# Linear attention and two feed-forward layers: the down, up and second down products as seven half-size block products each

## What is computed

```python
def _attn_ref(q, k, v):                       # q, k, v: (8, 8, 576, 64)
    q_s = softmax(q, axis=-1)                 # each with + 1e-09 under the sum
    k_s = softmax(k, axis=2)
    kv = np.einsum('bhsd,bhse->bhde', k_s, v)
    return np.einsum('bhsd,bhde->bhse', q_s, kv)

# x: attention's output as 4608 tokens x 512
def _moe_ref(x, w_gate, w_val, w_out):        # d_ff 1536
    g = x @ w_gate
    return (g * (1 / (1 + np.exp(-g))) * (x @ w_val)) @ w_out

def _moe2_ref(x, w_in, w_out):                # d_ff 2048; this w_out is w_out2 in the kernel
    h = x @ w_in
    g = np.where(h > 0.0, h, np.exp(np.minimum(h, 0.0)) - 1.0)
    return g @ w_out
```

## Time and profile before

| what | value |
|---|---|
| median of three runs | 1824.34 us |
| span of the profiled execution | 1820.5 us |
| TensorE busy | 1797.6 us, 99% of the span |
| VectorE busy | 763.9 us, 42% |
| ScalarE busy | 562.7 us, 31% |
| GpSimd busy | 131.6 us, 7% |
| mean granted TensorE clock | 0.998 of full speed |

### The profile page before, as it was taken

One profiled execution on the slowest core, in us unless ns is written; L12 is line 12 of the kernel. 1 busy time (PEld: TensorE's weight loads), 2 busy tenths in 40 slices (PEclk: granted clock), 3 DMA queues, 4 the chain that ended last, 5 costly groups with the idle time before them and its releaser, 6 DMA issues.

```text
span 1820.5 us, 21697 instructions
## 1 busy us (share of the span) xinstructions
PE 1797.6 (99%) x8156; PEld 1480.3 (81%) x8156; DVE 763.9 (42%) x1276; ACT 562.7 (31%) x846; POOL 131.6 (7%) x78
## 2 busy tenths in 40 slices
PE   7899999999999999999999999999999999999999
PEld 5688888888888888888888788888888888888887
DVE  6764544545355453542122434343434343433333
ACT  4333333333333333332121223232323232322222
POOL 6800000000000000000007400000000000000000
PEclk9999999999999999999999999999999999999999
DMA  7613121131311313112022301010101010101000
GB/s 216 171 34 95 55 78 50 34 94 55 95 34 34 94 55 101 27 34 76 1 73 89 115 1 46 0 46 0 46 0 46 0 46 0 46 0 46 0 23 23
DMA packets 122421, 94.67 MB, mean 52 GB/s; under 512 B 59936, under 2 KB 96800, under 8 KB 122400
## 3 DMA queue, kind: packets, MB, share of 16 engines
q1 hardware_dynamic: 113424, 76.57, 14.3%
q10 hardware_dynamic: 8976, 17.83, 2.8%
HBM read 66.06 MB, written 28.31 MB: 52 GB/s over the span
## 4 chain that ended last, share of the span: by engine, by line
PE 96%; DVE 3%; issue 1%; ACT 0%; SPq 0%; DMA 0%; DVEq 0%; ACTq 0%
PE psum L537 31%; PE psum L539 30%; PE psum L538 30%; PE psum L492 2%; PE psum L501 1%; PE psum L483 0%; DVE x_lo L812 0%; PE psum L502 0%; DVE k_rowmax L740 0%; DVE x_lo L829 0%; DVE hid_lo L848 0%; DVE q_negmax L746 0%; DVE hid L845 0%; DVE k L776 0%; ACT hid_hi L686 0%
## 5 line engine op out<-in xcount | busy, mean ns | idle before, releaser
L537 PE MATMUL psum<-x_hi,weights 128*128 128x512 f32 x1440 | 569.8, 396 | 5.6 <-DVE x_lo L812 3.5
L539 PE MATMUL psum<-x_lo,weights 128*128 128x512 f32 x1440 | 562.5, 391 | 0.0
L538 PE MATMUL psum<-x_hi,weights 128*128 128x512 f32 x1440 | 561.9, 390 | 0.0
L537 PEld LDWEIGHTS psum<-x_hi,weights 128*128 128x128 f32 x1440 | 271.1, 188 | 65.3 <-DVE x_lo L812 4.3
L539 PEld LDWEIGHTS psum<-x_lo,weights 128*128 128x128 f32 x1440 | 271.1, 188 | 57.6
L538 PEld LDWEIGHTS psum<-x_hi,weights 128*128 128x128 f32 x1440 | 271.3, 188 | 53.9
L537 PE MATMUL psum<-weights,hid_hi 128*128 128x512 f32 x576 | 224.1, 389 | 0.0
L538 PE MATMUL psum<-weights,hid_lo 128*128 128x512 f32 x576 | 224.1, 389 | 0.0
L539 PE MATMUL psum<-weights,hid_hi 128*128 128x512 f32 x576 | 224.1, 389 | 0.0
L845 DVE TENSOR_TENSOR hid<-psum,act_out 128x512 f32<-128x512 f32 x108 | 74.6, 691 | 351.4 <-PE psum L539 323.7
L862 DVE TENSOR_SCALAR act_out<-act_out 128x512 f32<-128x512 f32 x144 | 61.5, 427 | 362.9 <-ACT act_out L702 362.4
(11 more groups left out here) (75 smaller groups left out, 1467.9 us busy)
## 6 DMA issues: line engine op xcount, KB each, us to landing
attention_out_T<-ek_x SPq DMA_DIRECT2D x32, 288.0 KB, 2.2
layer_out_T<-stage ACTq DMA_DIRECT2D x9, 1024.0 KB, 5.0
stage<-layer_out_T SPq DMA_DIRECT2D x9, 1024.0 KB, 5.1
k<-in_k_dram SPq DMA_DIRECT2D x32, 256.0 KB, 2.7
q<-in_q_dram SPq DMA_DIRECT2D x32, 256.0 KB, 2.8
v<-in_v_dram SPq DMA_DIRECT2D x64, 128.0 KB, 2.8
stage<-attention_out_T SPq DMA_DIRECT2D x8, 1024.0 KB, 5.2
out_dram<-stage ACTq DMA_DIRECT2D x8, 1024.0 KB, 4.4
```

Of the source, the lines that this page charges most:

```text
L537: pe.matmul(acc, w_hi, xh, start=start, stop=False)
L538: pe.matmul(acc, w_lo, xh, start=False, stop=False)
L539: return pe.matmul(acc, w_hi, xl, start=False, stop=stop)
```

## The change

The program becomes four stages with their rows in DRAM between. Stage A is gate and value with attention, stage B is w_out, stage C is w_in, and stage D is w_out2. Stage A still works on nine chunks of 512 tokens, with 24 passes per tile and no down product; it stores the hidden rows. Attention's pairs are 6 slots apart instead of 7, and alternate between two pairs of banks.

Stages B, C and D cut weights and rows into 2x2 blocks and form each block product by seven products instead of eight, with added and subtracted blocks (the Winograd variant of Strassen's form: blocks A11, A12, A22 and sums S1 to S4 of the weights). The tokens go in five pairs of halves, of 480, 480, 448, 448 and 448 columns. Per pair B makes 7 forms x 2 output tiles x 6 contraction tiles x 3 passes = 252 passes, C makes 336 in four groups, and D makes 336. GpSimd makes the weight forms in 22 units during stage A, and stores them to DRAM, from which each stage loads its own. It also makes the sums of the rows in B and D (`sum_blocks`), and in C the sums and all `lo` halves of the rows (`split_y`). VectorE makes the `lo` halves in B and D, adds partial products (`add_parts`, `add_u`), does ELU in C (`elu`) and turns D's output in 32x32 blocks, which is then stored in runs of 128 bytes. A ring of 12 split tiles serves B (two forms of 6) and one of 8 serves D (one form of 8).

```diff
+    NX = 480
+    halves = [480, 480, 448, 448, 448]
+    pairs_of_tokens = []
+    at = 0
+    for n in halves:
+        pairs_of_tokens.append((at, n))
+        at += 2 * n
+    assert at == T and max(halves) == NX
+    NP = len(halves)
+    KT1, KT2, KTD = J1 // 2, J2 // 2, KD // 2
+    MW = DM // 2
...
+            def free_for(self, engine, p, i, kt):
+                t = self.seq(p, i, kt) - self.ring
+                if t >= 0:
+                    engine.wait_ge(self.p_done, t // self.kt * (self.kt + 1) + t % self.kt + 2)
...
+            for u in range(len(units)):
+                pool.wait_ge(fact_landed, (u + 1) * 64)
+                pool.tensor_tensor(form(F_S1), form(7), form(F_A22), ALU.add).then_inc(fact_step, 1)
+                pool.tensor_tensor(form(F_S3), form(F_A11), form(7), ALU.subtract).then_inc(fact_step, 1)
+                pool.wait_ge(fact_step, u * 5 + 1)
+                pool.tensor_tensor(form(F_S2), form(F_S1), form(F_A11), ALU.subtract).then_inc(fact_step, 1)
+                pool.wait_ge(fact_step, u * 5 + 3)
+                pool.tensor_tensor(form(F_S4), form(F_A12), form(F_S2), ALU.subtract).then_inc(fact_step, 1)
+                if u:
+                    pool.wait_ge(fact_stored, stores_of(u) * 16)
+                pool.wait_ge(fact_step, u * 5 + 4)
+                pool.tensor_scalar(fact_forms[:, 0, :, :], fact_raw[:, 0:7, :], 1.0, 1.0, ALU.mult, ALU.mult
+                                   ).then_inc(fact_step, 1)
+                pool.wait_ge(fact_step, u * 5 + 5)
+                pool.tensor_tensor(fact_forms[:, 1, :, :], fact_raw[:, 0:7, :], fact_forms[:, 0, :, :].bitcast(F32),
...
+            def sum_blocks(of, p):
+                _, n = pairs_of_tokens[p]
+                r11, r21, r12, r22 = of.slots(p)
+                def chunk(slot, c):
+                    return of.block(slot, n)[:, c * of.chunk:(c + 1) * of.chunk, :]
+                for c in range(of.chunks):
+                    pool.wait_ge(of.raw_landed[r11], 16 * (p + 1))
+                    pool.wait_ge(of.raw_landed[r12], 16 * (p + 1))
+                    pool.tensor_tensor(chunk(r12, c), chunk(r12, c), chunk(r11, c), ALU.subtract).then_inc(of.t_made, 1)
...
+                    pool.wait_ge(of.raw_landed[r22], 16 * (p + 1))
+                    pool.wait_ge(of.lo_made, of.seq(p, 3, (c + 1) * of.chunk - 1) + 1)
+                    pool.wait_ge(of.t_made, of.sums(p, 0, c))
+                    pool.tensor_tensor(chunk(r22, c), chunk(r22, c), chunk(r12, c), ALU.subtract).then_inc(of.t_made, 1)
...
+            def rest_of_y(p, i):
+                _, n = pairs_of_tokens[p]
+                pool.wait_ge(y_hi_made, 7 * p + i + 1)
+                pool.tensor_tensor(c_block(c_lo[i], n), y_source(p, i, n), c_block(c_hi[i], n).bitcast(F32),
+                                   ALU.subtract).then_inc(y_lo_made, 1)
+            def split_y(p):
+                sum_y(p, 0)
+                sum_y(p, 1)
+                rest_of_y(p, 0)
+                sum_y(p, 2)
+                rest_of_y(p, 1)
+                sum_y(p, 3)
+                for i in range(2, 7):
+                    rest_of_y(p, i)
+            for p in range(NP):
+                sum_blocks(stage_b, p)
+            for p in range(NP):
+                split_y(p)
+            for p in range(NP):
+                sum_blocks(stage_d, p)
...
+            def layer1(n):
...
+                    if n == 0:
+                        pe.wait_ge(w_split if j else w0_split, j if j else 1)
+                    if g >= 2:
+                        pe.wait_ge(silu_done, g - 1)
+                    into_hidden(GATE[g % 2], w_g, n, j == 0).then_inc(gate_done, 1)
+                    if n < BA:
                         attend(n, 3 * j)
-                    if j:
-                        pe.wait_ge(h_made, n * J1 + j)
-                    else:
+                    if g == 0:
                         pe.wait_ge(w0_split, 2)
-                    into_hidden(VAL, w_v, n, False).then_inc(val_done, 1)
-                    if with_attention:
+                    if g >= 2:
+                        pe.wait_ge(h_made, g - 1)
+                    into_hidden(VAL[g % 2], w_v, n, False).then_inc(val_done, 1)
+                    if n < BA:
                         attend(n, 3 * j + 1)
-                    if j:
...
+            def down(of, bank, p, i, dp):
+                _, n = pairs_of_tokens[p]
+                w = of.w[i]
+                for kt in range(of.kt):
+                    t = of.seq(p, i, kt)
+                    if dp == 0:
+                        pe.wait_ge(of.lo_made, t + 1)
+                    r = t % of.ring
+                    mm = product(psum[:, bank, 0:n], [w[:, half, kt, dp * P:(dp + 1) * P] for half in range(2)],
+                                 (of.hi[r][:, 0:n], of.lo[r][:, 0:n]),
+                                 kt == 0 and i in (0, 1, 2), kt == of.kt - 1, i > 2)
+                    if dp == 1 or kt == of.kt - 1:
+                        mm.then_inc(of.p_done, 1)
...
+                                    pe.wait_ge(*before[2][dp])
+                            elif i == 3:
+                                bank = 6 + dp
+                                pe.wait_ge(of.p5_copied, u + 1)
+                            else:
+                                bank = dp
+                                pe.wait_ge((of.p1_copied, of.c12_made, of.c22_made)[i - 4], u + 1)
+                            down(of, bank, p, i, dp)
...
+            def rest_of_tile(of, p, i, kt):
+                _, n = pairs_of_tokens[p]
+                t = of.seq(p, i, kt)
+                dve.wait_ge(of.hi_made, t + 1)
+                dve.tensor_tensor(of.lo[t % of.ring][:, 0:n], of.block(of.slot_of(p, i), n)[:, kt, :],
+                                  of.hi[t % of.ring][:, 0:n].bitcast(F32), ALU.subtract).then_inc(of.lo_made, 1)
+            def rest_of_form(of, f):
+                if f < 7 * NP:
+                    for kt in range(of.kt):
+                        rest_of_tile(of, f // 7, f % 7, kt)
...
+            def down_stage(of, part):
+                for f in range(7 * NP):
+                    p, i = divmod(f, 7)
+                    part(p, i, 0)
+                    rest_of_form(of, f + of.ahead)
+                    part(p, i, 1)
...
+            def elu(u, x, at, k):
...
+                e = c_e[x][f][:, side * n:side * n + n]
+                of = psum[:, c_bank(u, x), 0:n] if at == (1, 0) else c_s[x][{(0, 0): 0, (0, 1): 1, (1, 1): 2}[at]][:, 0:n]
+                dve.wait_ge(exped, 2 * u + x + 1)
+                dve.tensor_scalar(e, e, 1.0, 1.0, ALU.min, ALU.subtract).then_inc(m_made, 1)
+                dve.wait_ge(m_made, u * 8 + k + 1)
+                dve.scalar_tensor_tensor(out=e, in0=of, scalar=0.0, in1=e, op0=ALU.max, op1=ALU.add).then_inc(made, 1)
+            def up_stage():
+                for u in range(NP * NG):
+                    if u:
+                        elu(u - 1, 1, (1, 0), 7)
+                    add_u(u, 0, 1)
+                    add_u(u, 1, 1)
+                    elu(u, 0, (0, 0), 0)
+                    elu(u, 1, (0, 0), 1)
+                    add_u(u, 0, 4)
+                    add_u(u, 1, 4)
+                    elu(u, 0, (1, 1), 2)
```

More of the change, by code:

```diff
@@ L38, in attention_two_ffn_kernel @@
     CH = T // C
-    TB = C // P
     HP = H // 2
@@ new lines, in rest_of_x, with beside @@
+            def rest_of_x(n, kd):
+                dve.wait_ge(x_hi_made, n * KD + (kd + 1))
+                dve.tensor_tensor(x_lo[n % 2][:, kd, :], stage[:, kd, :], x_hi[n % 2][:, kd, :].bitcast(F32),
+                                  ALU.subtract).then_inc(x_lo_made, 1)
+            def beside(n, slot):
+                if n < BA:
+                    for hp, step in steps_at(slot - START, STRIDE, STEPS):
+                        for work in steps.get(step, ()):
+                            work(n + 1, hp, False)
+                if n + 1 < CH and slot in X_SLOTS:
+                    rest_of_x(n + 1, X_SLOTS.index(slot))
```

1081 lines of the change are left out of this document (783 added, 298 removed).

## The result

The changed kernel takes 1958.9 us (median of 4 runs, 1956.4 to 1962.0) against 1823.9 us for the kernel before in the same series (1821.9 to 1824.4): ratio 1.074, 95% interval 1.073 to 1.076. It is slower by 135 us, although 132 passes of TensorE are gone and 4620 others are narrower. The forecast was 1906 us, with a range of 1776 to 1985.

What follows compares the result with a forecast made beforehand. TensorE, busy 1797.6 of 1820.5 us, was taken as the bound; 131.4 us less of passes gave 1689.1, and + 50 + 8 + 35 + 24 + 70 + 9 + 17 = 1902.1 profiled, 1906 as median; range 1776 to 1985.

Steps and rivals of the forecast that it cites:

- Pace of the passes: TensorE: passes of 512, 480 and 448 columns take 0.2262, 0.2125 and 0.1987 us, together 131.4 us fewer.
- Stage A: 50 + 8 expected: Stage A: two TensorE waits for each of 28 pairs of heads, 50 us; GpSimd's weight units delaying VectorE, 8 us.
- The second wait: Stage A: turn_q directly behind sum_kv on TensorE waits for VectorE's k_den to kv, 1.2 us a pair of heads.
- The first: Stage A: spread_max directly behind turn_max on TensorE waits for VectorE's k_max, 0.6 us a pair of heads.
- B: 35 expected: Stage B: GpSimd's sums taking turns with VectorE's lo halves delay additions, 7 us a pair, 35 us (bounds 2 and 12 a pair).
- C: 24 expected: Stage C: GpSimd's nine instructions beside each last group delay VectorE, 6 us at each of four crossings, 24 us.
- D: 70 expected: Stage D: GpSimd's burst of sums slows the lo halves of form 4, 14 us a pair, 70 us (bounds 4 and 24).
- Hand-overs and clock: 9 + 17 expected: Three stage changes at 3 us each, 9 us; ten falls of TensorE's clock to 1.2 GHz at 1.7 us, 17 us.
- The base of 1689.1 us: Whole kernel: profiled time if nothing waited, 1820.5 us before less 131.4 us of passes.
- That the turns fit into gaps: Rival for B, C and D: GpSimd's and VectorE's turns mostly cost nothing, so the kernel is faster, 1784 us; chance 0.27.
- The pace set by something other than columns: Rival for TensorE: narrower passes still take 0.2262 us, only 30 us are saved, 2007 us; chance 0.02.
- the second rival: D, C and B at their upper bounds by late sums, 228 us instead of 129, so 2005 us; chance 0.11.

Runs made afterwards that it cites:

- the kernel with both repairs: Changed kernel with attention's second slot ahead of the value block and the sums of B and D made by VectorE: 1759.6 us, ratio 0.965.
- the fillers: Changed kernel with eight more TensorE passes, into a bank nobody reads, ahead of waits for lo tiles in D: 1945.2 us, ratio 1.067.

## Why the prediction was right in kind, and where its sizes were off

The sign and the mechanisms were right, the sum was 53 us short: 1954.7 us profiled against 1902.1. The measured 1958.9 lies in the forecast's 1835 to 1970, near its upper end, and D missed its own sign: 471.4 us where I had put 420 to 440. Step by step, with the stages' times of the profiled executions:

**Pace of the passes: 27 us too low.** This is the step "480 columns take 0.2125 us and 448 take 0.1987". TensorE's timeline of the kernel with VectorE's sums:

```profile
1699.82 0.36 PE L901 MATMUL psum<-g_hi,g_w 128*128 128x448 f32 x1
...
1701.86 0.36 PE L902 MATMUL psum<-g_lo,g_w 128*128 128x448 f32 x1
```

Ten intervals in 2.04 us: 0.204 each and not near the 0.199 that I had asked for; 60 passes of 480 columns from 1180.06 us on start 0.218 apart. D without waits is 353.9 us for 1680 passes, 0.2107 against my 0.2042: 11 us in D, 6 in B (263.1 for 257.3) and, at the same pace, 11 in C. From 512 down to 480 columns a column is worth 0.25 ns, from 480 to 448 0.44: the straight line through 288 and 512 columns gave too much for the first steps down. The Trainium skill's rule in the prediction ("TensorE: Matmul & The Clock Gate", Back-to-back issue gap) has a flatter one: N/2.4 + 2.5 gives 0.189 and 0.2025 us, both below the measured 0.204 and 0.218, so the trace does not bear out its level; its saving, an estimate of 126.9 us, was nearer to what these rows give (131.4 - 27, so about 104) than mine, though still above it.

**Stage A: 50 + 8 expected, 74 us measured** (770.5 against 696.1 without both causes): 62 us for the order of slots, about 9 for the units. The second wait was right: 32.9 / 28 = 1.2 us each, as worked out. The first was 31.1 / 31 = 1.0 rather than 0.6, and the step that failed is "VectorE multiplies `hid` just before, but does so under make_x or sum_kv". VectorE's timeline:

```profile
229.87 0.69 DVE L1445 TENSOR_TENSOR hid<-psum,act_out 128x512 f32<-128x512 f32 x1 [1.95 <-PE psum L933]
230.48 0.28 DVE L1358 TENSOR_REDUCE k_max<-psum 128x1 f32<-128x128 f32 x1
```

The transposition starts at 229.61 directly behind the value block, and so does `hid`; k_max stands behind it in VectorE's list and begins 0.6 us after the transposition has ended (229.61 + 0.27).

**B: 35 expected, 26.5 measured** (289.6 against 263.1 with VectorE's sums). **C: 24 expected, 32 measured** (386.0 against 354 at D's pace), but 10 of the 32 is the store behind the weight loads, which I had bounded as "at most 15 us at a hand-over" and not put in the sum. The crossings alone are then 22, close to my 24. C is not sharp to better than 10 us, but moving its sums to VectorE for the four crossings gave 20 us, which is the same within that.

**D: 70 expected, 117 measured** (471.4 against 353.9). By the starts of its passes, against the same forms in the kernel with sums of 2 elements, form 4 is 69.5 us longer over the five pairs, form 3 is 14.1, and forms 0 and 1 are 33.9. So form 4 alone took what I had given to all of D: 13.9 us a pair for my 14 (12.6 to 15.2). That this fits so well is in part luck. The period is 2.6 us and not 2.25 + 0.58 = 2.83, since a lo half adds 0.35 us to GpSimd's turn and not 0.58; and 2 of the 13.9 are slow passes, which I had counted apart. The step that failed is "The sums left over and the next pair's first sum fall mostly beside idle stretches of VectorE". The trace has, in each pair, gaps at tiles 5 and 7 of form 3, where the second sum alternates with the lo halves (0.75 and 1.5 to 1.6 us), and three more where the next first sum runs: at form 1 in the first pair (4.2 us together), at form 0 in the others (3.3 to 4.2). Without the clock's 13 to 21 us the turns cost 19 to 21 us a pair in place of 14, under my upper bound of 24.

**Hand-overs and clock: 9 + 17 expected.** They lie inside the stages' times above. The clock is 13 to 21 us in D, more than the 8.5 that my count of falls put there: each of the ten falls cost some 2.1 us behind its gaps, near my 1.7, but D has two a pair and not one. The total closes to 12 us: 27 + 16 - 8.5 + 8 + 47.5 - 26 is 64 for 52.6. The base of 1689.1 us explains a gap of this size: it was taken from the kernel before with waits of its own in it. Its view of waits has 19.5 us for TensorE, from k_max 4.8 down to qT 0.5, and of these releasers the kernel with weight units of 2 columns has 7.4 left. No run tests this.

**The rivals.** That the turns fit into gaps (1784 us) fell: the sums on GpSimd alone cost 135 us. The pace set by something other than columns fell too: 0.204 is not 0.226. Of the second rival only D came near: 117 us with the clock, where its bound was 120.

The Trainium skill's rule on VectorE ("VectorE: DVE Perf Modes", The DRAIN you can't avoid) would have each operation end before the next begins. Undisturbed, eight g_lo of 480 columns take 5.23 us, 0.654 each, with a mean of 0.654 in the group of the kernel with VectorE's sums. So for a lo half alone the rule's 0.65 was nearer than my 0.58; why the four x_lo of rows 10 took only 0.62 each no run shows. In the shared turn neither holds: there a lo half adds 0.35 us.

## What to carry to other kernels

Before work is given to an idle engine, ask whether it can run beside the one it is to relieve: here GpSimd spent 196 us on D's sums and lengthened VectorE's own work by 138, and VectorE made the same sums in 89 (52.2 and 36.9 us in its groups). Where such work must stay, make its instructions short: an instruction of the other engine waits for the length of one of them. And in a list that an engine works off in order, two steps with a round trip through another engine between them need other work between them; moving one call back in both engines' lists gave 62 us.

## What the runs showed of the hardware

An instruction of VectorE with its inputs in SBUF and one of GpSimd ran in turn, one for one, whether GpSimd's had one input or two: 2.62 us a lo half beside sums of 2.56, 1.37 beside copies of 1.29, 0.65 alone. The length of VectorE's own instruction does not set this: one cast of 128 elements (kv_hi at 239.16) took 2.37 us and ended 0.1 us behind the GpSimd instruction beside it. The mean of all 28 casts went from 246 ns in the kernel before to 1008, and it is 434 in the kernel with both repairs and 227 when there the weight units have 2 columns. The held engine is shown as busy.

The Trainium skill ("SBUF — State Buffer", SBUF: two separate sides) describes a port pair that the two engines share and that one of them holds for a whole instruction. It counts the operations of GpSimd, and on VectorE's side those in a two-port fast mode, and those with two SBUF inputs when GpSimd's operation reads SBUF. The runs agree in this: copies with one input held VectorE as subtractions did, and of VectorE's operations with one input the cast was held. Whether it ran in a fast mode no run shows.

A 32x32 block transposition of 480 columns takes 678 ns and of 448 takes 646, within the bounds of 0.28 and 0.69 and close to the 0.65 taken.

Passes at 1.2 GHz cost less than their extra busy time where waits follow: D had 49 us more busy time in its 1680 passes (402.8 against 353.9), and keeping the clock up gave 13, net of what the fillers cost.
